# Attention and gated MLP on one core: the last gate tile in three column parts, and a third staging buffer for the output

## The chip, the cores and the metric

The kernel runs on one core of a Trainium2 chip. The metric is the device time in microseconds from one execution of the whole program. The engines are TensorE (PE; its weight loads are listed apart as PEld), VectorE (DVE), ScalarE (ACT), GpSimd (POOL) and SyncE (SP), which here only issues DMAs. Each engine runs its own stream of instructions in order, and the streams meet in semaphores.

## The reference

```python
# q, k, v: (4, 8, 576, 64)   w_in: (512, 2048)   w_out: (2048, 512)   alpha: (2048,)
q_rot, k_rot = rotate(q), rotate(k)
scores = scale * np.matmul(q_rot, k_rot.transpose(0, 1, 3, 2))
attn = softmax(scores)
x = np.matmul(attn, v)            # -> 2304 tokens x 512
h = x @ w_in
g = np.maximum(h, 0.0) + alpha * np.minimum(h, 0.0)
return (g @ w_out).astype(np.float32)
```

## The kernel before

The program has two stages. First comes attention, in 16 periods (4 batches x 4 pairs of heads), which leaves x transposed in SBUF. Then comes the MLP over 2304 tokens in 6 chunks of 384 tokens (`CHUNK`). Each chunk is three blocks of 128 tokens (`MT`), and its hidden width of 2048 is cut into 16 tiles of 128 (`FT`, index f). The change touches the MLP stage only.

All matmuls of the MLP keep fp32 accuracy by splitting each operand into a high part and a low part and adding three products: high x high, high x low, low x high.

For one tile f of chunk (i, c), in this order:

- `hidden` on TensorE: 12 matmuls of 384 columns into one of two PSUM banks `h_ps[f % 2]`.
- `positive` on ScalarE (L808): `pos` = relu of the bank.
- `gate` on VectorE: `g` = alpha * min(h, 0) (L981, raises `neg_done`), then `g` += `pos` (L984, after a wait on `neg_done`, raises `g_done`). Columns are tokens, so the 384 columns are the three blocks of 128 tokens.
- `high` on ScalarE (L816): `g_hi` = `g` rounded, raises `g_hi_done`.
- `low` on GpSimd (L455): `g_lo` = `g` - `g_hi`, raises `g_lo_done`.
- `output` on TensorE (L656): waits for `g_lo_done`, then for each block m of 128 tokens three matmuls of 512 columns (g_hi x w_out_hi, g_hi x w_out_lo, g_lo x w_out_hi) that add to the PSUM bank of that block.

`g`, `g_hi`, `g_lo` and `pos` have two buffers each. TensorE issues `hidden` of tile f ahead of `output` of tile f - 1, so that everywhere but at the very end the gate of a tile runs beside the matmuls of its neighbours. After `hidden` of the last tile of the last chunk, TensorE has only `output` of tile 14 and then `output` of tile 15 left.

On the last tile, `output` raises `y_done` after blocks 0 and 1, and `g_used` at its end. `to_stage` on ScalarE (L828) then copies the bank of block m to `stage`, after a wait until the store that last read this buffer has landed (`stored`). SyncE issues one DMA of 128 x 512 values for each block (L362), 18 in the whole program, and at the end waits for all of them. There are two staging buffers, used in turn: block 0 of the last chunk goes to buffer 1, block 1 to buffer 0, block 2 to buffer 1 again. In the chunks before, the three copies are spread over tiles 1 to 3 of the next chunk.

`chunks` writes the first and the last chunk out and runs the four between in a loop of two iterations, so the last chunk has instructions of its own on each engine.

Of the kernel before, what the change touches and what calls it, by code (L numbers as in the profile page):

```python
# [6 lines left out]
F32 = mybir.dt.float32  # L7
F32R = mybir.dt.float32r
ALU = mybir.AluOpType
ACT = mybir.ActivationFunctionType  # L10
AX = mybir.AxisListType

P = 128
# [18 lines left out]
def build(nc, q, k, v, w_in, w_out, alpha, cos, sin, eye, out):  # L32
    NB, NH, S, D = q.shape
    DM, F = w_in.shape
# [7 lines left out]
    FT = F // P  # L42
    CHUNK = 384
    MT = CHUNK // P
    NCHUNK = TOK // CHUNK
# [49 lines left out]
    def evac_count(p, u):  # L95

        return tally(p, u, range(u % T_BANKS, UNITS, T_BANKS))
# [15 lines left out]
    with ExitStack() as ctx:  # L113
        used = [0]

        def sb(stack, name, shape, dt=F32):
            used[0] += -(-4 * int(np.prod(shape[1:])) // 32) * 32
            return stack.enter_context(nc.sbuf_tensor(name, shape, dt))

        def sem(name):  # L120
            return ctx.enter_context(nc.semaphore(name))
# [13 lines left out]
        alpha_sb = sb(ctx, "alpha_sb", [P, FT])  # L135
# [48 lines left out]
        pos = [sb(ctx, f"pos{i}", [P, CHUNK]) for i in range(2)]  # L184
# [3 lines left out]
        g = [sb(ctx, f"g{i}", [P, CHUNK]) for i in range(2)]  # L188
        g_hi = [sb(ctx, f"g_hi{i}", [P, CHUNK], F32R) for i in range(2)]
        g_lo = [sb(ctx, f"g_lo{i}", [P, CHUNK], F32R) for i in range(2)]  # L190
        assert used[0] <= until_prob + 8 * QT * S
        w_out_hi = sb(ctx, "w_out_hi", [P, FT, DM], F32R)
        x_lo[1] = sb(ctx, "x_lo1", [P, CT, CHUNK], F32R)
        stage = [sb(ctx, f"stage{i}", [P, DM]) for i in range(2)]
        if attention_bytes > used[0]:
            sb(ctx, "behind", [P, (attention_bytes - used[0]) // 4])

# [11 lines left out]
        h_ps = [banks[:, 0, 0:CHUNK], banks[:, 1, 0:CHUNK]]  # L209
        y_ps = [[banks[:, 2 + i, :] for i in range(MT)], [banks[:, 5 + i, :] for i in range(MT)]]  # L210
# [31 lines left out]
        neg_done = sem("neg_done")  # L242
        g_done = sem("g_done")
        g_hi_done = sem("g_hi_done")
        g_lo_done = sem("g_lo_done")
        g_used = sem("g_used")
        y_done = sem("y_done")
        staged = sem("staged")
        stored = [sem("stored0"), sem("stored1")]

        block = ctx.enter_context(nc.Block())

# [15 lines left out]
        def is_first(i, c):  # L268
            return isinstance(i, int) and i == 0 and c == 0

        def is_final(i, c):
            return isinstance(i, int) and i * 2 + c == NCHUNK - 1


        @block.sync
        def _(sp):
# [81 lines left out]
            def chunk(i, c):  # L358
                for m in range(MT):
                    n = (i * 2 + c) * MT + m  # L360
                    sp.wait_ge(staged, n + 1)
                    sp.dma_start(out[bass.ds(n * P, P), :], stage[(c * MT + m) % 2][:, :]).then_inc(  # L362
                        stored[(c * MT + m) % 2], 16)

            chunks(sp, chunk)
            for s in stored:
                sp.wait_ge(s, 16 * NCHUNK * MT // 2)


        @block.gpsimd  # L370
        def _(pool):
# [77 lines left out]
            def low(i, c, f):  # L449

                n = (i * 2 + c) * FT + f
                pool.wait_ge(g_hi_done, n + 1)
                if not (is_first(i, c) and f < 2):
                    pool.wait_ge(g_used, n - 1)
                nc.gpsimd.tensor_tensor(g_lo[f % 2][:, :], g[f % 2][:, :], g_hi[f % 2][:, :].bitcast(F32),  # L455
                                        ALU.subtract).then_inc(g_lo_done, 1)

            low(0, 0, 0)

            def chunk(i, c):  # L460
                for f in range(1 if is_first(i, c) else 0, FT):
                    low(i, c, f)
# [5 lines left out]
        def _(pe):  # L468
# [165 lines left out]
            def output(i, c, f):  # L634

                n = (i * 2 + c) * FT + f
                pe.wait_ge(g_lo_done, n + 1)
                if is_first(i, c):
                    pe.wait_ge(w_out_split, f + 1)
                elif c == 0:  # L640
                    pe.wait_ge(w_out_split, FT)
                if f == 0:
                    if is_first(i, c):
                        pe.wait_ge(exp_done, PERIODS * TILES)
                        pe.wait_ge(evac[U_PB[3] % T_BANKS], evac_count(PERIODS, U_PB[3]))
                    elif c == 2:
                        pe.wait_ge(staged, (i * 2 + c - 1) * MT)
                if c == 2 and f == FT // 2:
                    pe.wait_ge(staged, (i * 2 + c) * MT)
                for m in range(MT):  # L650
                    if f == FT - 1 and m:
                        mm.then_inc(y_done, 1)
                    lhs = (g_hi, g_hi, g_lo)
                    rhs = (w_out_hi, w_out_lo, w_out_hi)
                    for j in range(3):
                        mm = nc.tensor.matmul(y_ps[c % 2][m], lhs[j][f % 2][:, m * P:(m + 1) * P], rhs[j][:, f, :],  # L656
                                              start=(f == 0 and j == 0), stop=(f == FT - 1 and j == 2))
                mm.then_inc(g_used, 1)

            def chunk(i, c):  # L660

                for f in range(FT):
                    if not (is_first(i, c) and f < 2):
                        hidden(i, c, f)
                    if f:
                        output(i, c, f - 1)
                    elif not is_first(i, c):
                        output(i, c - 1, FT - 1)
                if is_final(i, c):
                    output(i, c, FT - 1)  # L670
# [16 lines left out]
        def _(act):  # L687
# [73 lines left out]
            def period(b, t):  # L761
# [20 lines left out]
                if not has_now(p):  # L782
                    positive(0, 0, 0)
                    high(0, 0, 0)
# [25 lines left out]
            def high(i, c, f):  # L810

                n = (i * 2 + c) * FT + f
                act.wait_ge(g_done, n + 1)
                if not (isinstance(n, int) and n < 2):
                    act.wait_ge(g_used, n - 1)
                nc.scalar.activation(g_hi[f % 2][:, :], g[f % 2][:, :], ACT.Copy).then_inc(g_hi_done, 1)  # L816

            def to_stage(i, c, m):

                n = (i * 2 + c) * MT + m  # L820
                if m < MT - 1:
                    act.wait_ge(y_done, (i * 2 + c) * (MT - 1) + m + 1)
                else:
                    act.wait_ge(g_used, (i * 2 + c + 1) * FT)
                before = i * MT + (c * MT + m) // 2
                if not (isinstance(before, int) and before == 0):
                    act.wait_ge(stored[(c * MT + m) % 2], before * 16)
                nc.scalar.activation(stage[(c * MT + m) % 2][:, :], y_ps[c % 2][m], ACT.Copy).then_inc(staged, 1)  # L828

            HEADS = (slice(0, D), slice(D, P))  # L830
            act.wait_ge(padded, PADDED)
# [12 lines left out]
            def chunk(i, c):  # L844
                for f in range(1 if is_first(i, c) else 0, FT):
                    positive(i, c, f)
                    if is_first(i, c):
                        high_w_out(f)
                    high(i, c, f)
                    if 1 <= f <= MT and not is_first(i, c):  # L850
                        to_stage(i, c - 1, f - 1)

            chunks(act, chunk)
            for m in range(MT):
                to_stage(NCHUNK // 2 - 1, 1, m)
# [3 lines left out]
        def _(dve):  # L859
# [115 lines left out]
            def gate(i, c, f):  # L975

                n = (i * 2 + c) * FT + f
                dve.wait_ge(pos_done, n + 1)
                if not (is_first(i, c) and f < 2):
                    dve.wait_ge(g_lo_done, n - 1)  # L980
                nc.vector.tensor_scalar(g[f % 2][:, :], h_ps[f % 2], 0.0, alpha_sb[:, f:f + 1],  # L981
                                        ALU.min, ALU.mult).then_inc(neg_done, 1)
                dve.wait_ge(neg_done, n + 1)
                nc.vector.tensor_tensor(g[f % 2][:, :], g[f % 2][:, :], pos[f % 2][:, :],  # L984
                                        ALU.add).then_inc(g_done, 1)

            def period(b, t):

# [28 lines left out]
                if not has_now(p):  # L1017
                    low_w_out(0)
                    dve.wait_ge(alpha_in, 16)
                    gate(0, 0, 0)  # L1020
# [34 lines left out]
            def chunk(i, c):  # L1055
                for f in range(FT):
                    if not (is_first(i, c) and f == 0):
                        gate(i, c, f)
                    if f in X_AT and not is_final(i, c):
                        split_x(i, c + 1, X_AT.index(f))  # L1060
                    if is_first(i, c):
                        if f:
                            low_w_out(f)
# [31 lines left out]
```

## Time and profile before

| | us |
|---|---|
| median of 3 runs | 699.22 (698.68 to 699.78) |
| the profiled execution, whole time | 698.69 |
| its span, first to last instruction | 696.9 |
| TensorE busy in the span | 676.4 (97%) |
| MLP stage in the span | from about 290 to the end |
| from the end of `hidden` of the last tile (686.6) to the end of the span | 10.3 |

The profile is of one execution. Its own time, 698.69 us, is 1.8 us more than its span and 0.53 us less than the median of the three runs. Times in rows count from the start of the span. TensorE's rows overlap, since a matmul starts while the one before drains; the distance from start to start is what a matmul costs in a row of them, and the length of one is what someone who waits for it sees.

### The profile page before, as it was taken

Reading aid. Unit: us, or ns where it says so; the run is one execution under the profiler, and the core shown is the slowest. Engines: PE = TensorE matmul, PEld = TensorE weight load, DVE = VectorE, ACT = ScalarE, POOL = GpSimd, SP = SyncE. Lnnn points to the kernel's source line nnn. Section 1 sums busy time; section 2 is a strip of 40 time slices with the busy share of each in tenths; the row PEclk is TensorE's granted clock in tenths of the full one; section 3 lists DMA queues with packets and bytes.
Section 4 is the critical chain, followed back from the end, with each engine's and each line's share of the span. In section 5 each row is a group of like instructions: output and inputs, shape, how many; then the busy total and the mean of one; then the engine's idle time right before and its main releaser. Section 6 shows DMA issues by size and latency. Waiting matters only on the chain.

```text
span 696.9 us, 12112 instructions
## 1 busy us (share of the span) xinstructions
PE 676.4 (97%) x4100; PEld 588.3 (84%) x4100; DVE 368.8 (53%) x677; ACT 316.2 (45%) x744; POOL 281.5 (40%) x258
## 2 busy tenths in 40 slices
PE   3899999999999999999999999999999999999996
PEld 2788888888888887698889999999999999999995
DVE  4688888888888887545542343233323323432231
ACT  2677777777777776433333223222222232223222
POOL 5656677777776503222222222222222222222221
PEclk9999999999999999999999999999999999999999
DMA  6898555666666643600001000000000010001001
GB/s 153 218 226 211 138 135 135 141 143 143 143 143 139 150 113 89 240 1 1 0 2 46 0 1 16 32 0 1 30 15 0 0 45 0 0 0 46 1 1 46
DMA packets 76619, 51.30 MB, mean 74 GB/s; under 512 B 61088, under 2 KB 61472, under 8 KB 76064
## 3 DMA queue, kind: packets, MB, share of 16 engines
q1 hardware_dynamic: 76576, 50.76, 29.0%
q8 instruction: 24, 0.39, 0.2%
q14 instruction: 19, 0.16, 0.1%
HBM read 22.95 MB, written 4.72 MB: 40 GB/s over the span
## 4 chain that ended last, share of the span: by engine, by line
PE 76%; issue 16%; POOL 2%; DVE 2%; DMA 1%; SPq 0%; ACT 0%; POOLq 0%; DVEq 0%; ACTq 0%
PE banks L629 19%; PE banks L656 19%; PE banks L553 14%; PE banks L511 12%; PE banks L575 10%; POOL g_lo L455 2%; PE banks L571 2%; DVE pt L916 0%; DMA k_two<-k_hi 0%; DMA raw_q<-in_q 0%; DVE nmax L867 0%; DMA out<-stage 0%; DVE k_lo L892 0%; DVE prob L1035 0%; ACT stage L828 0%
## 5 line engine op out<-in xcount | busy, mean ns | idle before, releaser
L455 POOL TENSOR_TENSOR g_lo<-g,g_hi 128x384 fp32r<-128x384 f32 x96 | 99.4, 1035 | 308.8 <-ACT g_hi L816 299.6
L981 DVE TENSOR_SCALAR g<-banks,alpha_sb 128x384 f32<-128x384 f32 x96 | 59.3, 618 | 250.9 <-ACT pos L808 250.9
L629 PE MATMUL banks<-x_hi,w_in_lo 128*128 128x384 f32 x384 | 129.5, 337 | 0.0
L629 PE MATMUL banks<-x_hi,w_in_hi 128*128 128x384 f32 x384 | 129.5, 337 | 0.0
L629 PE MATMUL banks<-x_lo,w_in_hi 128*128 128x384 f32 x384 | 129.2, 337 | 0.0
L808 ACT ACTIVATE pos<-banks 128x384 f32<-128x384 f32 x96 | 47.2, 491 | 170.2 <-PE banks L629 170.2
L867 DVE TENSOR_REDUCE nmax<-banks 128x1 f32<-128x576 f32 x144 | 108.7, 755 | 25.7 <-PE banks L511 20.7
L656 PE MATMUL banks<-w_out_hi,g_hi 128*128 128x512 f32 x288 | 114.9, 399 | 1.6 <-POOL g_lo L455 1.4
L656 PE MATMUL banks<-w_out_hi,g_lo 128*128 128x512 f32 x288 | 113.0, 392 | 0.0
L656 PE MATMUL banks<-w_out_lo,g_hi 128*128 128x512 f32 x288 | 112.1, 389 | 0.0
L816 ACT ACTIVATE g_hi<-g 128x384 fp32r<-128x384 f32 x96 | 50.4, 525 | 115.9 <-DVE g L984 115.9
L705 ACT ACTIVATE prob<-banks,nmax 128x576 f32<-128x576 f32 x128 | 94.8, 740 | 11.3 <-DVE nmax L867 8.2
L629 PEld LDWEIGHTS banks<-x_hi,w_in_hi 128*128 128x128 f32 x384 | 72.3, 188 | 4.5 <-issue 0.9
L553 PE MATMUL banks<-ident,prob 128*128 128x128 f32 x576 | 75.7, 273 | 0.0
L629 PEld LDWEIGHTS banks<-x_lo,w_in_hi 128*128 128x128 f32 x384 | 72.4, 188 | 3.5
L629 PEld LDWEIGHTS banks<-x_hi,w_in_lo 128*128 128x128 f32 x384 | 72.4, 188 | 0.0
L753 ACT ACTIVATE pt<-banks 128x512 f32<-128x512 f32 (+1 forms) x112 | 54.8, 490 | 35.4 <-PE banks L553 35.1
L575 PE MATMUL banks<-pt,raw_v 128*64 128x288 f32 x512 | 69.2, 413 | 0.0
L553 PEld LDWEIGHTS banks<-ident,prob 128*128 128x128 f32 x576 | 67.0, 141 | 0.3 <-issue 0.2
L511 PE MATMUL banks<-k_two,q_two 128*128 128x288 f32 x252 | 65.3, 341 | 1.9 <-DMA k_two<-k_hi 0.9
L656 PEld LDWEIGHTS banks<-w_out_hi,g_lo 128*128 128x128 f32 x288 | 54.0, 188 | 13.7
L656 PEld LDWEIGHTS banks<-w_out_hi,g_hi 128*128 128x128 f32 x288 | 54.1, 188 | 10.8 <-POOL g_lo L455 1.8
(85 smaller groups left out, 907.5 us busy)
## 6 DMA issues: line engine op xcount, KB each, us to landing
k_two<-k_hi SPq DMA_DIRECT2D x64, 160.0 KB, 2.9
out<-stage SPq DMA_DIRECT2D x18, 256.0 KB, 2.0
raw_q<-in_q SPq DMA_DIRECT2D x32, 128.0 KB, 2.7
raw_k<-in_k SPq DMA_DIRECT2D x32, 128.0 KB, 2.4
q_two<-q_hi SPq DMA_DIRECT2D x32, 128.0 KB, 2.3
q_two<-q_lo SPq DMA_DIRECT2D x32, 128.0 KB, 2.3
q_own<-q_hi SPq DMA_DIRECT2D x32, 128.0 KB, 2.4
raw_v<-in_v SPq DMA_DIRECT2D x32, 128.0 KB, 2.3
```

What stands on the lines that cost most here:

```text
L455: nc.gpsimd.tensor_tensor(g_lo[f % 2][:, :], g[f % 2][:, :], g_hi[f % 2][:, :].bitcast(F32), ALU.subtract).then_inc(g_lo_done, 1)
L511: mm = nc.tensor.matmul(tile[:, h, :], lhs[:, :], rhs[:, first + h * HALF:first + (h + 1) * HALF], start=(j == 0), stop=(j == len(products ...
L553: mm = nc.tensor.transpose(bank[:, i * P:(i + 1) * P], block_in, ident[:, :])
L575: mm = nc.tensor.matmul(o[own, :], raw_v[par][:, j, own], pt[:, pt_slot(par, head, j), cols], start=False, stop=(j == QT - 1))
L629: mm = nc.tensor.matmul(h_ps[f % 2], w[:, j, cols], xx[:, j, :], start=(step == 0), stop=(step == 3 * CT - 1))
L656: mm = nc.tensor.matmul(y_ps[c % 2][m], lhs[j][f % 2][:, m * P:(m + 1) * P], rhs[j][:, f, :], start=(f == 0 and j == 0), stop=(f == FT - 1 ...
L705: nc.scalar.activation(dst.rearrange("p (h s) -> p h s", h=2), s_ps[(t * TILES + n) % 2], ACT.Exp, bias=nmax[:, t % 2, n:n + 1], accum_out ...
L753: ins = nc.scalar.activation(dst, src, ACT.Copy)
L808: nc.scalar.activation(pos[f % 2][:, :], h_ps[f % 2], ACT.Relu).then_inc(pos_done, 1)
L816: nc.scalar.activation(g_hi[f % 2][:, :], g[f % 2][:, :], ACT.Copy).then_inc(g_hi_done, 1)
L867: nc.vector.tensor_reduce(nmax[:, t % 2, n:n + 1], s_ps[(t * TILES + n) % 2], AX.XY, ALU.max, negate=True).then_inc(max_done, 1)
L981: nc.vector.tensor_scalar(g[f % 2][:, :], h_ps[f % 2], 0.0, alpha_sb[:, f:f + 1], ALU.min, ALU.mult).then_inc(neg_done, 1)
```

## The change

It does three things.

- `parts` gives three column parts of 128 for the last tile of the last chunk, and one part of 384 for all others. `gate`, `high` and `low` run over the parts, with the semaphores counted up by one for each part.
- `output` of that one tile waits for `g_lo_done` once more ahead of block 1 and ahead of block 2.
- `stage` and `stored` have three buffers and three semaphores, one for each block m.

```diff
-        stage = [sb(ctx, f"stage{i}", [P, DM]) for i in range(2)]
+        stage = [sb(ctx, f"stage{i}", [P, DM]) for i in range(MT)]
...
-        stored = [sem("stored0"), sem("stored1")]
+        stored = [sem(f"stored{i}") for i in range(MT)]
...
+        def parts(i, c, f):
+
+            if is_final(i, c) and f == FT - 1:
+                return [slice(m * P, (m + 1) * P) for m in range(MT)]
+            return [slice(0, CHUNK)]
...
-                    sp.dma_start(out[bass.ds(n * P, P), :], stage[(c * MT + m) % 2][:, :]).then_inc(
-                        stored[(c * MT + m) % 2], 16)
+                    sp.dma_start(out[bass.ds(n * P, P), :], stage[m][:, :]).then_inc(stored[m], 16)
...
+                for m, part in enumerate(parts(i, c, f)):
+                    pool.wait_ge(g_hi_done, n + 1 + m)
+                    if m == 0 and not (is_first(i, c) and f < 2):
+                        pool.wait_ge(g_used, n - 1)
+                    nc.gpsimd.tensor_tensor(g_lo[f % 2][:, part], g[f % 2][:, part], g_hi[f % 2][:, part].bitcast(F32),
+                                            ALU.subtract).then_inc(g_lo_done, 1)
...
                 for m in range(MT):
+                    if m and len(parts(i, c, f)) > 1:
+                        pe.wait_ge(g_lo_done, n + 1 + m)
...
+                for m, part in enumerate(parts(i, c, f)):
+                    act.wait_ge(g_done, n + 1 + m)
+                    if m == 0 and not (isinstance(n, int) and n < 2):
+                        act.wait_ge(g_used, n - 1)
+                    nc.scalar.activation(g_hi[f % 2][:, part], g[f % 2][:, part], ACT.Copy).then_inc(g_hi_done, 1)
...
-                before = i * MT + (c * MT + m) // 2
-                if not (isinstance(before, int) and before == 0):
-                    act.wait_ge(stored[(c * MT + m) % 2], before * 16)
-                nc.scalar.activation(stage[(c * MT + m) % 2][:, :], y_ps[c % 2][m], ACT.Copy).then_inc(staged, 1)
+                if not is_first(i, c):
+                    act.wait_ge(stored[m], (i * 2 + c) * 16)
+                nc.scalar.activation(stage[m][:, :], y_ps[c % 2][m], ACT.Copy).then_inc(staged, 1)
...
+                for m, part in enumerate(parts(i, c, f)):
+                    nc.vector.tensor_scalar(g[f % 2][:, part], h_ps[f % 2][:, part], 0.0, alpha_sb[:, f:f + 1],
+                                            ALU.min, ALU.mult).then_inc(neg_done, 1)
+                    dve.wait_ge(neg_done, n + 1 + m)
+                    nc.vector.tensor_tensor(g[f % 2][:, part], g[f % 2][:, part], pos[f % 2][:, part],
+                                            ALU.add).then_inc(g_done, 1)
```

On VectorE the end of the program is the gate of tiles 14 and 15 of the last chunk. Before, by line, operation, operands (number of the buffer behind the name), size and the semaphores waited for:

```order
L984 TENSOR_TENSOR g1<-g1,pos1 128x384 [waits neg_done]
L981 TENSOR_SCALAR g0<-banks,alpha_sb 128x384 [waits g_lo_done,pos_done]
L984 TENSOR_TENSOR g0<-g0,pos0 128x384 [waits neg_done]
L981 TENSOR_SCALAR g1<-banks,alpha_sb 128x384 [waits g_lo_done,pos_done]
L984 TENSOR_TENSOR g1<-g1,pos1 128x384 [waits neg_done]
```

The same place on VectorE after the change:

```order
L990 TENSOR_SCALAR g0<-banks,alpha_sb 128x384 [waits g_lo_done,pos_done]
L993 TENSOR_TENSOR g0<-g0,pos0 128x384 [waits neg_done]
L990 TENSOR_SCALAR g1<-banks,alpha_sb 128x128 [waits g_lo_done,pos_done]
L993 TENSOR_TENSOR g1<-g1,pos1 128x128 [waits neg_done]
L990 TENSOR_SCALAR g1<-banks,alpha_sb 128x128
L993 TENSOR_TENSOR g1<-g1,pos1 128x128 [waits neg_done]
L990 TENSOR_SCALAR g1<-banks,alpha_sb 128x128
L993 TENSOR_TENSOR g1<-g1,pos1 128x128 [waits neg_done]
```

The last two instructions became six of a third of the width, a minimum and an addition in turn.

On ScalarE the end of the program is `pos` and `g_hi` of the last two tiles and the three copies to `stage`. Before:

```order
L808 ACTIVATE pos0<-banks 128x384 [waits g_done,h_done]
L816 ACTIVATE g_hi0<-g0 128x384 [waits g_used,g_done]
L808 ACTIVATE pos1<-banks 128x384 [waits g_done,h_done]
L816 ACTIVATE g_hi1<-g1 128x384 [waits g_used,g_done]
L828 ACTIVATE stage1<-banks 128x512 [waits stored1,y_done]
L828 ACTIVATE stage0<-banks 128x512 [waits stored0,y_done]
L828 ACTIVATE stage1<-banks 128x512 [waits stored1,g_used]
```

And after the change:

```order
L825 ACTIVATE g_hi0<-g0 128x384 [waits g_used,g_done]
L816 ACTIVATE pos1<-banks 128x384 [waits g_done,h_done]
L825 ACTIVATE g_hi1<-g1 128x128 [waits g_used,g_done]
L825 ACTIVATE g_hi1<-g1 128x128 [waits g_done] x2
L836 ACTIVATE stage0<-banks 128x512 [waits stored0,y_done]
L836 ACTIVATE stage1<-banks 128x512 [waits stored1,y_done]
L836 ACTIVATE stage2<-banks 128x512 [waits stored2,g_used]
```

The rounding of the last tile is three instructions, and the last copy goes to a buffer of its own, whose semaphore was raised last by the chunk before.

## Rows read from the trace of the kernel before

**Rows 1.** The page: span, busy time of each engine, granted TensorE clock.

```profile
span 696.9 us, 12112 instructions
...
PE 676.4 (97%) x4100; PEld 588.3 (84%) x4100; DVE 368.8 (53%) x677; ACT 316.2 (45%) x744; POOL 281.5 (40%) x258
...
PEclk9999999999999999999999999999999999999999
```

**Rows 2.** Timeline of the end: start, length (us), engine, line, operation, [idle before, releaser].

```profile
686.29 0.34 PE L629 MATMUL banks<-x_hi,w_in_lo 128*128 128x384 f32 x1
...
686.67 0.49 ACT L808 ACTIVATE pos<-banks 128x384 f32<-128x384 f32 x1 [1.87 <-PE banks L629]
...
687.19 0.62 DVE L981 TENSOR_SCALAR g<-banks,alpha_sb 128x384 f32<-128x384 f32 x1 [2.95 <-ACT pos L808]
...
687.85 0.56 DVE L984 TENSOR_TENSOR g<-g,pos 128x384 f32<-128x384 f32 x1
...
688.32 0.39 PE L656 MATMUL banks<-w_out_hi,g_lo 128*128 128x512 f32 x1
688.44 0.52 ACT L816 ACTIVATE g_hi<-g 128x384 fp32r<-128x384 f32 x1 [1.28 <-DVE g L984]
689.04 0.99 POOL L455 TENSOR_TENSOR g_lo<-g,g_hi 128x384 fp32r<-128x384 f32 x1 [3.14 <-ACT g_hi L816]
...
690.08 0.50 PE L656 MATMUL banks<-w_out_hi,g_hi 128*128 128x512 f32 x1 [1.38 <-POOL g_lo L455]
...
690.42 0.39 PE L656 MATMUL banks<-w_out_lo,g_hi 128*128 128x512 f32 x1
...
691.08 1.29 ACT L828 ACTIVATE stage<-banks 128x512 f32<-128x512 f32 x2 [2.12 <-PE banks L656]
...
692.04 0.40 PE L656 MATMUL banks<-w_out_hi,g_lo 128*128 128x512 f32 x1
693.83 0.60 ACT L828 ACTIVATE stage<-banks 128x512 f32<-128x512 f32 x1 [1.46 <-DMA out<-stage]
```

**Rows 3.** The last chain in order of time: start, length (us), what.

```profile
691.70 2.04 DMA out<-stage
```

**Rows 4.** Groups by shape, GpSimd, VectorE, ScalarE: shapes, count, busy us, mean ns.

```profile
L455 POOL TENSOR_TENSOR g_lo<-g,g_hi 128x384 fp32r<-128x384 f32 x96 | 99.4, 1035 | 308.8 <-ACT g_hi L816 299.6 <-PE banks L656 9.2
L385 POOL TENSOR_TENSOR swapped<-raw_k,sin_sb 128x320 f32<-128x320 f32 x30 | 25.5, 870 | 0.9
...
L407 POOL TENSOR_TENSOR w_in_lo<-w_in_raw,w_in_hi 128x512 fp32r<-128x512 f32 x4 | 5.1, 1278 | 0.3
...
L892 DVE TENSOR_TENSOR k_lo<-banks,k_hi 128x128 fp32r<-128x128 f32 x16 | 4.7, 292 | 0.2
...
L726 ACT ACTIVATE k_hi<-banks 128x128 fp32r<-128x128 f32 x16 | 4.4, 278 | 0.2
L734 ACT ACTIVATE prob_rem<-prob_rem 128x64 f32<-128x64 f32 x16 | 4.0, 248 | 0.0
```

**Rows 5.** Timeline of chunk 0 where VectorE and GpSimd meet, and once apart.

```profile
325.67 0.56 DVE L966 TENSOR_TENSOR x_lo<-x,x_hi 128x384 fp32r<-128x384 f32 x1
...
326.00 1.11 POOL L455 TENSOR_TENSOR g_lo<-g,g_hi 128x384 fp32r<-128x384 f32 x1 [3.14 <-ACT g_hi L816]
...
326.15 1.51 DVE L972 TENSOR_TENSOR w_out_lo<-w_out_raw,w_out_hi 128x512 fp32r<-128x512 f32 x1
...
329.44 0.69 DVE L972 TENSOR_TENSOR w_out_lo<-w_out_raw,w_out_hi 128x512 fp32r<-128x512 f32 x1
```

**Rows 6.** DMA engines' load in 40 slices of 691.5 to 694.5 (tenths busy).

```profile
DMA  0000000000000079999998999989989961000000
```

**Rows 7.** The same of 694 to 696.9.

```profile
DMA  1000000000000000049889999964000000000000
```

**Rows 8.** Waits by the engine named last: us in total, times, longest.

```profile
PEld banks L575 <- issue: 12.3, 32, 0.4
...
ACT stage L828 <- DMA out<-stage: 1.5, 1, 1.5
```

More of the change, by code:

```diff
@@ L361, in chunk @@
                     sp.wait_ge(staged, n + 1)
-                    sp.dma_start(out[bass.ds(n * P, P), :], stage[(c * MT + m) % 2][:, :]).then_inc(
-                        stored[(c * MT + m) % 2], 16)
+                    sp.dma_start(out[bass.ds(n * P, P), :], stage[m][:, :]).then_inc(stored[m], 16)
             chunks(sp, chunk)
             for s in stored:
-                sp.wait_ge(s, 16 * NCHUNK * MT // 2)
+                sp.wait_ge(s, 16 * NCHUNK)
         @block.gpsimd
@@ L451, in low @@
                 n = (i * 2 + c) * FT + f
[L452 to L456, printed above, removed]
+                for m, part in enumerate(parts(i, c, f)):
[4 more added lines that the diff above has]
+                                            ALU.subtract).then_inc(g_lo_done, 1)
             low(0, 0, 0)
@@ L812, in high @@
                 n = (i * 2 + c) * FT + f
[L813 to L816, printed above, removed]
+                for m, part in enumerate(parts(i, c, f)):
[3 more added lines that the diff above has]
+                    nc.scalar.activation(g_hi[f % 2][:, part], g[f % 2][:, part], ACT.Copy).then_inc(g_hi_done, 1)
             def to_stage(i, c, m):
@@ L980, in gate @@
                     dve.wait_ge(g_lo_done, n - 1)
[L981 to L985, printed above, removed]
+                for m, part in enumerate(parts(i, c, f)):
[4 more added lines that the diff above has]
+                                            ALU.add).then_inc(g_done, 1)
             def period(b, t):
```

## The prediction

> **What bounds the kernel now.** I read the page first, then the timeline of the end, then the prices by shape. TensorE is busy for 676.4 of 696.9 us at a granted clock of full speed throughout [rows 1], so 2.4 GHz. The change takes no matmul away, so it can only bring what the end of the program loses. There the timeline is one chain. `hidden` of the last tile ends at 686.63; then pos 686.67, minimum 687.19, addition 687.85, g_hi 688.44, g_lo 689.04 to 690.03 [rows 2]. TensorE had run out of other work at 688.71 (688.32 + 0.39) and starts the last `output` at 690.08: 1.38 us idle. Its nine matmuls start 0.34 us apart at first and then about 0.23, the last at 692.04, done at 692.44. The copy of block 2 could start at 692.46, and starts at 693.83, because its buffer is still being read by the store issued at 691.70, which takes 2.04 us [rows 2, 3]. That is 1.37 us. So two stalls stand one behind the other on the last chain, 1.38 and 1.37 us, together 2.75. The first is not wholly removable: block 2 must pass through the same four engines.
>
> **Third buffer.** In the chunks before, no copy ever waited for a store: the wait occurs once in 18 copies, and costs 1.5 us by that view, 1.37 behind the end of the matmuls [rows 8, 2]. The previous user of buffer 2 is a store of the chunk before, over 60 us old. So this part gives 1.37 us, if the last matmul stays where it is. What is late next is the last matmul itself, and ScalarE's copies of blocks 0 and 1 (0.60 + 0.69 from start to start).
>
> **Parts: the price of a piece.** The trace has no 128-column form of these four operations, so each is bounded from both sides.
> - GpSimd: 320 columns take 870 ns, 384 take about 1,017 (992 to 1,112; 1,035 the mean with the disturbed ones), 512 take 1,278 [rows 4]. That is (1278 - 1017) / 128 = 2.04 ns a column, so 128 columns are 1017 - 522 = 495 ns. The low end is a third, 340 ns, the high end the nearest row as it is, 870. I take 490, by the line through three sizes.
> - VectorE addition: the 128x128 subtraction takes 292 ns [rows 4]; I take 290. The minimum is 60 ns dearer than the addition at 384 columns (0.62 against 0.56 [rows 2]), so 350. The low ends are 190 and 210, a third of the whole.
> - ScalarE: 128 columns from PSUM 278 ns, 64 columns from SBUF 248 [rows 4], 384 from SBUF 520 [rows 2]. The line between the last two gives 303; I take 310, with 180 (a third) and 520 as ends.
> - Handing on, as in the chain now [rows 2]: 0.03 VectorE to itself and to ScalarE, 0.08 ScalarE to GpSimd, 0.05 GpSimd to TensorE. A VectorE instruction that waits for nothing starts about 0.08 before the end of the one before it (325.67 to 326.15 for a length of 0.56 [rows 5]).
>
> **The chain in parts**, from the same 687.19. Nothing up to `pos` changes.
> - VectorE: minimum 687.19 to .54, addition 687.57 to .86; second pair 687.78 to .13 and 688.16 to .45; third 688.37 to .72 and 688.75 to 689.04.
> - ScalarE: 687.89 to 688.20; 688.48 to .79; 689.07 to .38. Behind these on ScalarE are only the copies, the first due at 689.8, so the three waits hold up nobody.
> - GpSimd: 688.28 to .77; 688.87 to 689.36; 689.46 to .95. So g_lo is ready for TensorE at 688.82, 689.41 and 690.00.
> - TensorE: free at 688.71, starts at 688.82. The nine matmuls keep their pace now: block 1 can start at 688.82 + 0.34 + 2 x 0.23 = 689.62 (ready 689.41), block 2 at 690.31 (ready 690.00). The two added waits are met 0.2 and 0.3 us early and I cost them at nothing; if one is not met, the delay and a restart of about 0.11 (0.34 - 0.23) come on top. The last matmul starts at 688.82 + 1.96 = 690.78 and ends at 691.18.
> - ScalarE copies: 689.81 to 690.42 and 690.51 to 691.12; the third can start at 691.20. It started at 693.83. The sum of both parts is 2.63 us, 1.37 from the buffer and 1.26 from the parts.
>
> VectorE does 6 instructions for 2 (1.92 for 1.18 us of work), and GpSimd 3 for 1 (1.47 for 0.99). This is all in the open, but the first third arrives 1.26 us sooner, and that alone is what TensorE waits for.
>
> **What takes from it: VectorE and GpSimd meet.** In the chain now they take turns; in parts they overlap. The additions read two operands in SBUF (g and pos), and so does GpSimd. Rows show what that does: a VectorE subtraction that starts 0.15 after GpSimd's took 1.51 us instead of 0.69, and ended 0.55 after GpSimd's; and GpSimd's own, begun while a VectorE subtraction was running, took 1.11 against 1.02 [rows 5, 4]. Here the first g_lo (due 688.28) begins inside the second addition (688.16 to .45), and so it grows by about 0.1. The third addition (due 688.75) falls on its last 0.1 us and can finish by 0.15 after it, which is inside its own 0.29. The second g_lo (due 688.87) falls into the third addition and grows by 0.1, within the slack of 0.2. On the path, 0.10. The Trainium skill, in "SBUF — State Buffer", section "SBUF: two separate sides", calls the pair of ports an exclusive lock: who comes first holds it for the whole instruction, and the other fully blocks. By that, the first g_lo would start at 688.45, 0.17 late instead of 0.10, and the third addition and g_lo would be 0.2 to 0.3 late, which block 2 can just bear; the sum would be 0.07 us poorer. The 1.51 us of the trace agree with it better than with a shared rate.
>
> **Three stores at once.** A store moves data for about 0.8 us (11 to 12 slices of 0.07 [rows 7]). Two issued 0.69 us apart keep the DMA engines busy for about 20 slices of 0.075 = 1.5 to 1.6 us without a gap [rows 6]. So each store behind another is late by about 0.8 - 0.69 = 0.11. Before, the third went alone. Now it is third in such a row: issued at 691.82, late by some 0.2. Bounds: 0, and 0.5 if the landing also stretches.
>
> **Sum.** 2.63 - 0.10 - 0.20 = 2.33 us. Against its own execution: 698.69 - 2.33 = 696.36. The median of the runs was 0.53 higher, so I put the median after at 699.22 - 2.33 = 696.9.
>
> **Rivals.**
> - Pieces of GpSimd cost nearly a whole: at 870 ns, three in a row are 688.28 to 690.89, block 2 starts at 690.94, the last matmul ends at 691.94 (0.34 + 0.23 + 0.40 and a little), copy at 691.95: 1.88 - 0.2 = 1.6 to 1.7 us of gain, 697.6. For: the 320-column row is as near as the trace gets. Against: three sizes lie on one line.
> - The parts bring nothing, as if `output` still began with the third g_lo. Then only the buffer counts, and TensorE starts at 690.00 as against 690.08 now: 1.37 + 0.08 - 0.2 = 1.25 gained, 698.0, which is no change by my bound. It needs the order of waits to be otherwise than the listing has it, or a g_lo of over 1 us a piece.
> - Slower: the text of the program has changed on four engines, and TensorE waits for nothing visible ("issue") 32 times, 12.3 us in total, ahead of L575, 0.38 each [rows 8]. If the changed layout gave TensorE more such holes, 6 would eat the gain (2.33 / 0.38) and 10 would make the kernel slower by more than 0.2%: 700.7. Nothing on TensorE's stream changes but two waits at its very end, and therefore this is small.
> - The full price of everything at its low end (pieces of a third, no queueing of stores, no meeting): TensorE could not start before 688.71, which is 0.11 sooner and saves the restart of 0.11: 2.63 + 0.22 = 2.85 of gain, 696.4.
>
> **How the numbers follow.** A measurement of this kernel tells a change of about 0.2%, 1.4 us. Chances: the forecast (gain 2.0 to 2.7) 0.70, its cheap end (over 2.7) 0.07, dear pieces or slow stores (1.4 to 2.0) 0.12, parts without effect or other small gains (about 1.2) 0.08, slower 0.03. The forecast alone spans 696.5 to 697.2; the bounds of the prices widen it to 696.4 and 697.8, and three runs of before lie 1.1 us apart, so a median can be off by 0.4: 695.9 to 698.0. Faster by over 0.2% has 0.70 + 0.07 + 0.12 = 0.89, within 0.2% 0.08, slower 0.03.
>
> **What would show it.** In the profile after, the last `output` should start at 688.8 to 689.0 on the scale of before (1.6 to 1.8 us after the first minimum of the last tile), the pieces take 0.35, 0.29, 0.31 and 0.49 us, with the first g_lo a little longer; ahead of blocks 1 and 2 no idle time on TensorE; the third copy starts within 0.03 us of the last matmul's end and no longer behind a store; the third store lands 2.2 us after its issue. The prediction is wrong if a g_lo piece takes 0.7 us or more, if the third addition or g_lo is held over 0.4 us by the other engine, if three stores together take over 0.5 us longer than spaced, or if something ahead of 686.6 moves.

## The result, and the profile after

The kernel after the change takes 695.77 us (median of 21 runs), the kernel before 698.44 (median of 21). The ratio is 0.9966, with a 95% interval of 0.9956 to 0.9977: 0.34% faster, 2.4 us by the ratio and 2.7 by the medians. Four of the 21 runs after the change lie 2.6 to 4.2 us above their median, at a mean granted clock of 0.995 to 0.998, and none of the 21 before by more than 1.4. The profiled execution has a span of 693.9 us against 696.9.

The timeline of the end after the change, all engines, answers to [rows 2] (start, length in us, engine, line, operation, idle before and releaser):

```profile
686.20 0.49 ACT L816 ACTIVATE pos<-banks 128x384 f32<-128x384 f32 x1 [1.87 <-PE banks L635]
...
686.72 0.35 DVE L990 TENSOR_SCALAR g<-banks,alpha_sb 128x128 f32<-128x128 f32 x1 [2.95 <-ACT pos L816]
...
687.11 0.29 DVE L993 TENSOR_TENSOR g<-g,pos 128x128 f32<-128x128 f32 x1
...
687.43 0.31 ACT L825 ACTIVATE g_hi<-g 128x128 fp32r<-128x128 f32 x1 [0.74 <-DVE g L993]
...
687.69 0.29 DVE L993 TENSOR_TENSOR g<-g,pos 128x128 f32<-128x128 f32 x1
687.82 1.63 POOL L461 TENSOR_TENSOR g_lo<-g,g_hi 128x128 fp32r<-128x128 f32 x3 [2.40 <-ACT g_hi L825]
687.85 0.39 PE L664 MATMUL banks<-w_out_hi,g_lo 128*128 128x512 f32 x1
...
688.36 0.50 PE L664 MATMUL banks<-w_out_hi,g_hi 128*128 128x512 f32 x1
...
689.17 0.40 PE L664 MATMUL banks<-w_out_hi,g_hi 128*128 128x512 f32 x1
...
689.37 1.98 ACT L836 ACTIVATE stage<-banks 128x512 f32<-128x512 f32 x3 [0.45 <-PE banks L664]
...
689.87 0.39 PE L664 MATMUL banks<-w_out_hi,g_hi 128*128 128x512 f32 x1
...
690.32 0.39 PE L664 MATMUL banks<-w_out_hi,g_lo 128*128 128x512 f32 x1
```

The three pieces of GpSimd stand in one row, of 1.63 us; asked for one by one, they start at 687.82, 688.41 and 689.00 and take 0.48, 0.48 and 0.46. Tile 14's last matmul drains at 688.24 and the last `output` starts at 688.36, where TensorE had stood idle for 1.38 us [rows 2]. Blocks 1 and 2 start at 689.17 and 689.87, at the pace of matmuls that wait for nothing. The three copies run without a break.

The piece prices, from the groups by shape (shapes, count, busy us, mean ns), answer to [rows 4]:

```profile
L461 POOL TENSOR_TENSOR g_lo<-g,g_hi 128x128 fp32r<-128x128 f32 x3 | 1.4, 475 | 2.6 <-ACT g_hi L825 2.4
L990 DVE TENSOR_SCALAR g<-banks,alpha_sb 128x128 f32<-128x128 f32 x3 | 1.0, 346 | 2.9 <-ACT pos L816 2.9
L993 DVE TENSOR_TENSOR g<-g,pos 128x128 f32<-128x128 f32 x3 | 0.9, 293 | 0.1
L825 ACT ACTIVATE g_hi<-g 128x128 fp32r<-128x128 f32 x3 | 0.9, 310 | 1.3 <-DVE g L993 1.3
```

And the end of the chain in order of time (start, us, what), which answers to [rows 3]: between the last matmul and the third copy no store stands any more.

```profile
688.36 2.37 PE banks L664 x9
690.73 0.02 issue
690.75 0.60 ACT stage L836
```

The place to compare two executions is the first minimum of the last tile, since what lies ahead of it scatters. It stood at 687.19 before and at 686.72 after, although all that the change touches in front of it is which staging buffer a copy uses, and no copy waited there in either. In the nine profiles of the experiments it lies between 686.54 and 687.40, with no order that follows the edits. From that minimum on:

| | first `output` matmul of tile 15 | its last matmul starts | third copy starts | end of span |
|---|---|---|---|---|
| before | +2.89 | +4.85 | +6.64 | +9.7 |
| after | +1.64 | +3.60 | +4.03 | +7.2 |

So the end of the program is 2.5 us shorter. The other 0.5 us between the two spans of 696.9 and 693.9 lies ahead of that point. It is put down to scatter, since the nine profiles differ by up to 0.9 us there; of the kernel before there is only one profile.

### The profile page after: what moved, and what is told of

It is laid out like the page before. It is cut to its first block, busy times and chain, and to the rows that moved or that the text cites. A ratio compares the mean times of both kernels' runs of the same rounds, so it can differ in the third digit from the quotient of the medians.

```text
span 693.9 us, 12120 instructions
## 1 busy us (share of the span) xinstructions
PE 676.6 (98%) x4100; PEld 588.2 (85%) x4100; DVE 369.5 (53%) x681; ACT 316.6 (46%) x746; POOL 281.9 (41%) x260
## 4 chain that ended last, share of the span: by engine, by line
PE 95%; DVE 2%; SPq 1%; DMA 1%; issue 0%; ACT 0%; POOL 0%; DVEq 0%
PE banks L635 29%; PE banks L664 29%; PE banks L559 14%; PE banks L517 11%; PE banks L581 10%; PE banks L577 2%; DMA k_two<-k_hi 1%; SPq L306 0%; DVE nmax L875 0%; DMA raw_q<-in_q 0%; SPq L307 0%; DVE pt L924 0%; SPq L291 0%; DVE prob L1044 0%; SPq L309 0%
## 5 line engine op out<-in xcount | busy, mean ns | idle before, releaser
L461 POOL TENSOR_TENSOR g_lo<-g,g_hi 128x384 fp32r<-128x384 f32 (+1 forms) x98 | 99.8, 1018 | 308.9 <-ACT g_hi L825 305.6
L990 DVE TENSOR_SCALAR g<-banks,alpha_sb 128x384 f32<-128x384 f32 (+1 forms) x98 | 59.8, 610 | 250.9 <-ACT pos L816 250.9
L825 ACT ACTIVATE g_hi<-g 128x384 fp32r<-128x384 f32 (+1 forms) x98 | 50.9, 519 | 116.0 <-DVE g L993 116.0
```

What stands on the lines that cost most here:

```text
L461: nc.gpsimd.tensor_tensor(g_lo[f % 2][:, part], g[f % 2][:, part], g_hi[f % 2][:, part].bitcast(F32), ALU.subtract).then_inc(g_lo_done, 1)
L825: nc.scalar.activation(g_hi[f % 2][:, part], g[f % 2][:, part], ACT.Copy).then_inc(g_hi_done, 1)
L990: nc.vector.tensor_scalar(g[f % 2][:, part], h_ps[f % 2][:, part], 0.0, alpha_sb[:, f:f + 1], ALU.min, ALU.mult).then_inc(neg_done, 1)
```

## The experiments

All have the full change as their base unless it is said otherwise.

**One part alone.** First the buffer without the parts:

```diff
-            if is_final(i, c) and f == FT - 1:
+            if False:
                 return [slice(m * P, (m + 1) * P) for m in range(MT)]
```

> Third staging buffer, gate of the last tile in one piece. Theory (two stalls one behind the other, each removed by one part): the last output still starts 2.89 us after the first minimum of the last tile, the third copy starts within 0.03 us of the last matmul, 1.37 us sooner than before; less up to 0.1 us for three stores in a row. Time 1.3 us below before (ratio 0.9981), 1.25 us above the full change. Rival (the buffer wait was hidden anyway, all of the gain is the parts'): no change against before.

Measured: 697.28 us, ratio 0.998 (0.997 to 0.9989) against before. The first row below is the start of the last `output`, 2.89 us after the first minimum (687.35), as before. The middle row shows the three copies in one run, so the third starts at 691.26 + 1.39 = 692.65, where the last matmul is over at 692.61.

```profile
690.24 0.50 PE L664 MATMUL banks<-w_out_hi,g_hi 128*128 128x512 f32 x1 [1.38 <-POOL g_lo L461]
...
691.26 1.99 ACT L836 ACTIVATE stage<-banks 128x512 f32<-128x512 f32 x3 [2.14 <-PE banks L664]
...
692.22 0.39 PE L664 MATMUL banks<-w_out_hi,g_lo 128*128 128x512 f32 x1
```

Then the parts with the two staging buffers of before:

```diff
-        stage = [sb(ctx, f"stage{i}", [P, DM]) for i in range(MT)]
+        stage = [sb(ctx, f"stage{i}", [P, DM]) for i in range(2)]
...
-                if not is_first(i, c):
-                    act.wait_ge(stored[m], (i * 2 + c) * 16)
-                nc.scalar.activation(stage[m][:, :], y_ps[c % 2][m], ACT.Copy).then_inc(staged, 1)
+                before = i * MT + (c * MT + m) // 2
+                if not (isinstance(before, int) and before == 0):
+                    act.wait_ge(stored[(c * MT + m) % 2], before * 16)
+                nc.scalar.activation(stage[(c * MT + m) % 2][:, :], y_ps[c % 2][m], ACT.Copy).then_inc(staged, 1)
```

> Gate of the last tile in three parts, two staging buffers. Theory: the last output starts 1.64 us after the first minimum instead of 2.89; block 0 is copied and stored 1.25 us sooner, so the store that the third copy waits for also lands 1.25 us sooner. The wait of the third copy stays at 1.4 to 1.5 us, and the time is 1.25 us below before (ratio 0.9982). Rival (the parts are swallowed by the buffer wait): the wait grows to 2.7 us and the time is that of before. That can't be unless the store of block 0 keeps its old place.

Measured: 697.42 us, ratio 0.9983 (0.9974 to 0.9993). The last `output` starts 1.63 us after the first minimum (687.36), and the wait for the store is as long as before [rows 2, 8]:

```profile
688.99 0.50 PE L665 MATMUL banks<-w_out_hi,g_hi 128*128 128x512 f32 x1
...
692.73 0.60 ACT L838 ACTIVATE stage<-banks 128x512 f32<-128x512 f32 x1 [1.45 <-DMA out<-stage]
```

The end lies 8.4 us after the first minimum in both, 1.3 less than before. The two gains, 0.20% and 0.17%, add up to 0.37% for the 0.34% of the full change, each with an interval of about 0.1% to either side; the profiles show the sum more sharply, 1.3 and 1.3 us for 2.5. Neither part covers the other: the store that the third copy waited for is moved by the parts together with everything else.

**Two parts in place of three.** Blocks 1 and 2 wait for one piece of 256 columns.

```diff
-                return [slice(m * P, (m + 1) * P) for m in range(MT)]
+                return [slice(0, P), slice(P, CHUNK)]
...
-                    if m and len(parts(i, c, f)) > 1:
+                    if m == 1 and len(parts(i, c, f)) > 1:
```

> Gate of the last tile in two parts, 128 and 256 columns, three staging buffers; blocks 1 and 2 both wait for the second part. Theory (the chain of pieces, by a fixed price and a price per column of each engine): the second g_lo takes about 0.75 us and ends about 2.8 us after the first minimum, where block 1 is due after 2.35; TensorE stands idle about 0.4 to 0.6 us ahead of block 1, and the time is 0.5 us above the full change, some 2.1 us below before (0.9970). Rival (only the first piece counts, what follows is hidden): the same time as the full change.

Measured: 696.77 us, ratio 0.9973 (0.9963 to 0.9983), 1.0 us above the full change, 0.75 above the repeat of the full change further down (696.02). Against the runs of before in its own set (698.60) it is 1.8 us faster, where 2.1 was expected. The timeline:

```profile
687.20 0.35 DVE L990 TENSOR_SCALAR g<-banks,alpha_sb 128x128 f32<-128x128 f32 x1 [2.95 <-ACT pos L816]
...
688.30 0.46 POOL L461 TENSOR_TENSOR g_lo<-g,g_hi 128x128 fp32r<-128x128 f32 x1 [2.40 <-ACT g_hi L825]
688.30 0.73 DVE L993 TENSOR_TENSOR g<-g,pos 128x256 f32<-128x256 f32 x1
...
689.57 0.72 POOL L461 TENSOR_TENSOR g_lo<-g,g_hi 128x256 fp32r<-128x256 f32 x1 [0.81 <-ACT g_hi L825]
...
690.34 0.50 PE L664 MATMUL banks<-w_out_hi,g_hi 128*128 128x512 f32 x1 [0.57 <-POOL g_lo L461]
```

The prices of the pieces hold (GpSimd 0.72 us for 256 columns), and the hole ahead of block 1 is there, 0.57 us. What the expectation missed is the second addition. Between 293 ns for 128 columns and 559 for 384 lie 426 for 256, and it took 0.73. It and GpSimd's first piece began together at 688.30, and it ended 0.27 us after GpSimd's. So the second g_lo was ready 3.09 us after the first minimum and not 2.8, and 0.3 us of the loss is the meeting of the two engines. With it the loss is 0.7 to 0.8 us, for the 0.5 expected.

**What a meeting costs.** Two kernels ask this directly, each with one more VectorE instruction behind the last addition, on data that nobody uses.

```diff
+                if len(parts(i, c, f)) > 1:
+                    nc.vector.tensor_tensor(x[:, 0:2, CHUNK:2 * CHUNK], x[:, 1:3, 0:CHUNK], x[:, 0:2, 0:CHUNK], ALU.add)
```

> The full change, and behind the last addition VectorE does one more addition of 2x384 columns, both operands in SBUF, result not used. It starts about 0.2 us after the start of the last addition, takes about 0.95 us, and is still running when the third g_lo is due, 0.5 us later. Exclusive theory: the third g_lo (0.46 us alone) is held until the addition is over and shows about 0.8 us or starts so much later; TensorE can just bear it. Sharing theory: it grows by less than 0.2 us.

Both were run once, 696.65 us for this one and 695.48 for the next, and are read by their profiles alone. Its timeline (the second row is GpSimd's second piece, asked for by itself, the fourth its third):

```profile
688.96 0.29 DVE L993 TENSOR_TENSOR g<-g,pos 128x128 f32<-128x128 f32 x1
...
689.08 0.48 POOL L461 TENSOR_TENSOR g_lo<-g,g_hi 128x128 fp32r<-128x128 f32 x1
...
689.17 1.22 DVE L996 TENSOR_TENSOR x<-x 128x768 f32<-128x768 f32 x1
...
689.67 1.03 POOL L461 TENSOR_TENSOR g_lo<-g,g_hi 128x128 fp32r<-128x128 f32 x1
...
690.76 0.51 PE L664 MATMUL banks<-w_out_hi,g_hi 128*128 128x512 f32 x1
```

The other differs in one operand, which comes from PSUM:

```diff
+                    nc.vector.tensor_tensor(x[:, 0:2, CHUNK:2 * CHUNK], banks[:, 0:2, 0:CHUNK], x[:, 0:2, 0:CHUNK], ALU.add)
```

> The same as the kernel with one more addition, but its first operand is the two PSUM banks of h, so that only one operand is in SBUF. Exclusive theory (only two operands in SBUF meet GpSimd): third g_lo 0.46 to 0.48 us, as in the full change. Rival (any VectorE work beside GpSimd slows it): the third g_lo is as long as with two operands in SBUF.

```profile
687.64 1.64 POOL L461 TENSOR_TENSOR g_lo<-g,g_hi 128x128 fp32r<-128x128 f32 x3 [2.40 <-ACT g_hi L825]
...
688.32 0.95 DVE L996 TENSOR_TENSOR x<-banks,x 128x768 f32<-128x768 f32 x1
```

With one operand in SBUF, the addition takes 0.95 us and GpSimd's three pieces 1.64, as in the full change. With two, the addition takes 1.22, GpSimd's third piece 1.03 where 0.46 was seen alone, and it ends (690.70) 0.31 us after the addition (690.39). The hold was longer than the 0.8 us expected, and it fell on the path, which was not expected: block 2 starts 0.92 us after block 1 (689.84) instead of 0.70. The sharing theory, with growth under 0.2, is out, and so is the rival in which any VectorE work beside GpSimd slows it. The exclusive theory stands in both directions, with one correction. In each meeting of over 0.1 us in the MLP stage of these traces the instruction that started second ends after the first one by its own length less 0.13 to 0.16 us (us, taken from the starts and lengths; "alone" is its length where it met nobody, for 256 and 768 columns by the line through 293 ns for 128 and 559 for 384, which for 768 agrees with the 0.95 above):

| started second | alone | ends after the other |
|---|---|---|
| first and second piece after the change, GpSimd 128 columns | 0.46 | 0.32 |
| third piece behind the addition of 768 columns | 0.46 | 0.31 |
| `g_lo` of a whole tile in chunk 0 [rows 5] | 1.02 | 0.88 |
| VectorE, 256 columns, kernel with two parts | 0.43 | 0.27 |
| VectorE, 512 columns, chunk 0 [rows 5] | 0.69 | 0.55 |
| VectorE, 768 columns | 0.95 | 0.82 |

So the first 0.14 us or so of the second instruction can run beside the other, and all the rest waits. That is worked out from these rows; what fills those 0.14 us is not shown.

**The last store alone.** The stores of blocks 0 and 1 of the last chunk are left out, so this kernel leaves 256 rows of the output unwritten; it was run once (695.93 us).

```diff
                     sp.wait_ge(staged, n + 1)
+                    if is_final(i, c) and m < MT - 1:
+                        continue
...
-            for s in stored:
-                sp.wait_ge(s, 16 * NCHUNK)
+            for m, s in enumerate(stored):
+                sp.wait_ge(s, 16 * (NCHUNK - (m < MT - 1)))
```

> The full change, but the stores of blocks 0 and 1 of the last chunk are left out, so 256 rows of the output are not written; the last store has the DMA engines to itself. Queueing theory: span from the start of the third copy to its end 0.08 us shorter than in the full change (3.15 us there, 3.07 in the kernel before, whose last store was alone too). Rival (the 0.08 us is scatter of a landing): 3.15 again.

The span is given to 0.1 us, which is too coarse for the 0.08 that was asked about. The DMA engines' load in slices of 0.06 us from the issue of the last store tells more. First this kernel (from 691.67), then the full change (from 691.37):

```profile
DMA  0000000000000079899988978710000000000000
```

```profile
DMA  8969979999998999899899989830000000000000
```

The load ends in the 27th slice in both, 1.6 us after the issue. Two stores in front of it do not delay the third by as much as a slice. The same view before the change, from 694.45, ends in the 27th slice too. The landings agree: by the semaphore events of the traces the last store lands 2.05 us after its issue in the full change, 2.01 with its two predecessors left out, and 2.00 before, where it went alone. So the delay is at most 0.05 us.

**A step further.** To see how good the end can get, the full change was run again beside two kernels that go on from it.

> The full change as it is, beside the next two kernels on the same chip: 2.4 to 2.7 us below before (ratio 0.9962 to 0.9966). From the first minimum of the last tile to the end of the span 7.2 us.

Measured: 696.02 us, ratio 0.9958 (0.9943 to 0.9974).

In the first, `output` of the last tile waits only for g_hi ahead of its first two products of a block:

```diff
-                pe.wait_ge(g_lo_done, n + 1)
+                split = len(parts(i, c, f)) > 1
+                pe.wait_ge(g_hi_done if split else g_lo_done, n + 1)
...
-                    if m and len(parts(i, c, f)) > 1:
-                        pe.wait_ge(g_lo_done, n + 1 + m)
+                    if m and split:
+                        pe.wait_ge(g_hi_done, n + 1 + m)
...
                     for j in range(3):
+                        if split and j == 2:
+                            pe.wait_ge(g_lo_done, n + 1 + m)
```

> In the last output each block waits for its g_hi, does its two g_hi products, and waits for g_lo only ahead of the third product. Theory (TensorE's last hole is the wait for the first g_lo): g_hi of block 0 is there before tile 14's last matmul is over, the hole of 0.12 us and the slow restart of 0.11 go, and the end comes 0.2 us sooner than in the full change: 7.0 us from the first minimum to the end. Rival (the three waits inside a block cost more than the hole): the same or later, with matmuls of the last tile more than 0.24 us apart.

Measured: 695.85 us, ratio 0.9967 (0.9947 to 0.9987); against the full change in the same set the medians differ by 0.17 us, less than they scatter, and by the ratios it would even be the slower one (0.9967 for 0.9958), because three of its eight runs lie over 1 us above the median. So the runs show no gain. The timeline is clearer, at the seam of tiles 14 and 15 and at the end:

```profile
687.12 0.35 DVE L993 TENSOR_SCALAR g<-banks,alpha_sb 128x128 f32<-128x128 f32 x1 [2.95 <-ACT pos L819]
...
688.24 0.39 PE L667 MATMUL banks<-w_out_hi,g_lo 128*128 128x512 f32 x1
...
688.47 0.39 PE L667 MATMUL banks<-w_out_hi,g_hi 128*128 128x512 f32 x1
...
690.32 0.39 PE L667 MATMUL banks<-w_out_hi,g_lo 128*128 128x512 f32 x1
```

Tile 15 follows tile 14 after 0.23 us, as any matmul follows another, and the last matmul starts 3.20 us after the first minimum instead of 3.60. That is 0.40, twice what was expected. A hole of 0.12 behind the drained matmul is 0.28 from start to start (688.36 - 687.85 = 0.51 against 0.23), and the slow restart is another 0.11. The end comes 6.8 us after the first minimum instead of 7.2. The six waits of the tile cost nothing that can be seen: its matmuls start 0.22 to 0.24 us apart.

The second also copies and stores block 2 in two halves:

```diff
+        def pieces(i, c, m):
+
+            if is_final(i, c) and m == MT - 1:
+                return [slice(0, DM // 2), slice(DM // 2, DM)]
+            return [slice(0, DM)]
...
+                for cols in pieces(i, c, m):
+                    nc.scalar.activation(stage[m][:, cols], y_ps[c % 2][m][:, cols], ACT.Copy).then_inc(staged, 1)
...
+                    for k, cols in enumerate(pieces(i, c, m)):
+                        sp.wait_ge(staged, n + 1 + k)
+                        sp.dma_start(out[bass.ds(n * P, P), cols], stage[m][:, cols]).then_inc(
+                            stored_half if k else stored[m], 16)
```

> As the kernel with the g_hi products first, and block 2 is copied and stored in two halves of 256 columns. Theory (what is left behind the last matmul is copy 0.60, issue to landing 2.04, of which about 0.8 us is data): two copies of about 0.39 us in a row end 0.18 us later than one, but the last store moves half the bytes, 0.4 us less of data. The end 0.1 to 0.2 us sooner than with the g_hi products first. Rival (a store costs its fixed time, or smaller packets move slower): the end 0.15 to 0.2 us later.

Measured: 695.75 us, ratio 0.9954 (0.9938 to 0.9969). The end is 6.8 us after the first minimum (686.87 to 693.7), which is the kernel without halves within the 0.1 of a span. Neither the gain nor the loss that was expected shows, and the trace says why. The copies cost little: they start at 690.50 and 690.78 and take 0.38 each, so the second ends 0.06 us later than one copy of 0.60 would. But SyncE is busy issuing the first half from 690.91 to 691.27 and issues the second at 691.32, 0.16 us behind its copy, where the kernel without halves issues 0.03 behind. Counted from the first minimum, the last issue is 0.20 us later (4.45 for 4.25). The half store then lands 1.91 us after its issue instead of 2.04. What remains is 0.07 us of loss in these two profiles. By their medians the two variants are 0.2 and 0.3 us below the full change and can't be told apart from it by the runs alone.

## Why the prediction was right

The forecast of 2.33 us less was close (2.4 by the ratio, 2.5 by the end of the profile). Its steps one by one:

- **Two stalls in a row, each removed by its own part.** Right, and shown by the two parts alone: 1.3 us each, neither hiding the other. The rival in which the parts bring nothing asked for 1.25 us in all and is out.
- **Prices of the pieces.** GpSimd 475 ns (taken 490), minimum 346 (350), addition 293 (290), ScalarE 310 (310). The line through the three sizes of GpSimd was the decisive choice, and the 256-column piece at 0.72 us lies near it too (756 ns by the line). It put the pieces 0.02 to 0.03 us too high. The rival with 870 ns a piece is out.
- **The chain.** The last `output` starts 1.64 us after the first minimum; the working had 1.63 without the meeting of the engines and 1.73 with it. Blocks 1 and 2 did not wait. The last matmul starts 1.96 us after the first, to the hundredth.
- **Meeting of VectorE and GpSimd, 0.10 on the path.** Oversized: the first piece began 0.13 us into the addition (687.69) and shows 0.48, against 0.46 for the third, which met nobody; 0.02. The working took the growth of [rows 5], 1.11 for 1.02, as it was; but there the overlap was 0.23 us, which is 0.09 more than the 0.14 that cost nothing, and here it was 0.17. The mechanism is real, and the experiments put it at 0.3 to 0.6 us where the order is unlucky. The rule of the Trainium skill, in "SBUF — State Buffer", section "SBUF: two separate sides", that the loser fully blocks while the other holds the ports for its whole instruction, would have started that piece at the addition's end, at 687.98, and finished it some 0.15 later than it did. Here the trace goes against the letter of it: the two overlapped for 0.16 us, nearly without cost. Where the overlap is longer the trace agrees with the rule up to the same 0.14 us, 1.22 us for 0.95 and 1.03 for 0.46.
- **Third store late by 0.20.** Wrong: at most 0.05 us. The store was to land 2.2 us after its issue and landed after 2.05, against 2.01 with its two predecessors left out. The step that failed is 0.8 - 0.69 = 0.11 us for each store in front, which made a queue of an overlap. The busy stretch of two stores in [rows 6], 1.5 to 1.6 us, is what two stores of 0.8 us started 0.69 apart fill without any delay, 0.69 + 0.8 = 1.49.
- **The level.** The two oversized terms, by 0.08 and by about 0.15 to 0.20 us, left the forecast 0.2 short of the profile's 2.5. So the forecast hit by the two stalls, 2.63 us by the working and 2.61 by the start of the third copy (6.64 less 4.03), and not by errors that cancelled: both erred to the same side. Most of the rest of the distance between 696.9 and 695.77 is the base: the median of before from three runs was 699.22, from 21 it is 698.44, 0.78 lower. So 695.77 itself lies 0.13 below the low end of the range; on the base that the prediction was made from, the measured ratio gives 699.22 x 0.9966 = 696.8. The allowance of 0.4 for the error of a median of three was too small, and it was not added in full either: 0.4 beyond the bounds of 696.4 and 697.8 is 696.0 to 698.2, not 695.9 to 698.0.
- **Slower through holes in TensorE's stream.** Did not happen. The view of waits after the change has the same hole as [rows 8], to the digit:

```profile
PEld banks L581 <- issue: 12.3, 32, 0.4
```

## What to carry to other kernels

At the end of a program nothing covers anything, so follow the last chain instruction by instruction and cut each link to the size that the next one consumes; a chain of four engines in three parts costs more work in total (1.92 us of VectorE for 1.18) and still ends sooner. Price a smaller piece by a line through several sizes of the same operation, not by a share of one. Count a buffer's wait separately from the work that feeds it: if both lie on the same chain, their savings add. When parts of a chain begin to overlap, check which engines had been taking turns until then: here the same idea in two parts instead of three ran into VectorE and GpSimd starting together.

## What the runs showed of the hardware that was not expected

- A VectorE addition with two SBUF operands and a GpSimd subtraction exclude each other but for the first 0.14 us or so of the later one, so that a tenth of a microsecond decides: the addition started 0.13 us before GpSimd's piece and both ran at nearly their own length (0.29 and 0.48); started at the same time, the addition of 256 columns took 0.73 instead of 0.43; started 0.09 after, one of 768 columns took 1.22 instead of 0.95, and the GpSimd piece that came next 1.03 instead of 0.46.
- A TensorE hole of 0.12 us, seen from the drained matmul to the next start, cost 0.39 us from start to start: 0.28 to the start, and 0.11 for a second matmul that follows after 0.34 and not 0.23.
- Three stores of 256 KB, issued 0.69 us apart, hardly delayed each other, although the 16 DMA engines were busy without a gap: the third landed after 2.05 us, and after 2.00 to 2.01 where it went alone.
- Issuing a store keeps SyncE busy for 0.33 to 0.45 us, so a store cut in two halves starts its second half late: 0.16 us behind its copy, where a whole one started 0.03 behind.
